# Rows gathered per job by a slot table instead of scattered, and job 0 fixed to expert 0

## The reference

```python
def reference(...):
    x = attn(q, k, v, g_q, g_k)       # batch 4, 12 heads, 448 rows, head width 64; q and k rms-normed
    x = x.transpose(0, 2, 1, 3).reshape(1792, 768)
    xn = x / (norm(x) + 1e-6)
    en = emb / (norm(emb) + 1e-6)
    logits = xn @ en.T / tau          # 8 experts
    expert = argmax(logits, 1)
    gate = softmax(logits)[expert]
    for e in range(8):                # w1: 768 x 1024, w2: 1024 x 768 per expert
        m = expert == e
        y[m] = gate[m, None] * (relu(x[m] @ w1[e]) @ w2[e])
    return (sigmoid(y @ w_gate) * (y @ w_val)) @ w_out    # 768 x 1536, 1536 x 768
```

## Time and profile before

| | us |
|---|---|
| median of 3 runs (1240.18 to 1243.33) | 1241.68 |
| the profiled execution | 1241.44 |
| its span, first to last instruction | 1239.7 |
| TensorE (PE) busy | 1136.6 (92%) |
| VectorE (DVE) busy | 650.4 (52%) |
| ScalarE (ACT) busy | 575.0 (46%) |
| GpSimd (POOL) busy | 238.3 (19%) |
| DMA moved | 146.28 MB, mean 118 GB/s |

### The profile page before, as it was taken

How to read it: one execution, slowest core, us unless ns; L and a number is a source line. 1 busy time by engine, 2 the same in 40 slices (tenths; PEclk the granted TensorE clock), 3 DMA queues, 4 the chain that set the end, 5 groups by cost and what they waited for, 6 DMA issues and landing times. The chain is left out here.

```text
span 1239.7 us, 22058 instructions
## 1 busy us (share of the span) xinstructions
PE 1136.6 (92%) x7426; PEld 997.4 (80%) x7427; DVE 650.4 (52%) x1112; ACT 575.0 (46%) x1272; POOL 238.3 (19%) x217
## 2 busy tenths in 40 slices
PE   4999999999406999999999899999999999999995
PEld 2566666666206999999999899999999999999995
DVE  4677777776625656666566333334433333334332
ACT  3777777777004555555555333233332433233321
POOL 7576766664330000000000000010000000010001
PEclk9999999999657999999999999999999999999998
DMA  2122121212177875778765643343333533343331
GB/s 88 28 66 61 50 67 44 67 45 53 35 202 188 204 188 160 184 194 232 194 171 167 157 120 108 102 147 102 103 112 96 156 110 102 102 146 102 111 111 50
DMA packets 242678, 146.28 MB, mean 118 GB/s; under 512 B 8258, under 2 KB 237890, under 8 KB 242574
## 3 DMA queue, kind: packets, MB, share of 16 engines
q1 hardware_dynamic: 240087, 134.86, 40.1%
q0 software_dynamic: 2560, 11.02, 2.7%
HBM read 133.94 MB, written 11.92 MB: 118 GB/s over the span
## 5 line engine op out<-in xcount | busy, mean ns | idle before, releaser
L1309 POOL DMA_INDIRECT out_dram<-rows,idp x16 | 18.2, 1136 | 861.3 <-DVE rows L1271 857.6
L1262 DVE TENSOR_TENSOR gv<-vb,sg 128x448 f32<-128x448 f32 x48 | 30.0, 625 | 218.4 <-PE vb L1327 218.4
L495 ACT ACTIVATE PR<-sc,negmax 112x448 f32<-112x448 f32 x192 | 122.2, 660 | 0.0
L1104 PE MATMUL hb<-XL,W1H 128*128 128x256 f32 (+1 forms) x384 | 110.1, 287 | 7.4 <-issue 7.4
L363 DVE TENSOR_REDUCE negmax<-sc 112x2 f32<-112x896 f32 x96 | 100.8, 1087 | 28.8 <-PE sc L590 28.6
L1103 PE MATMUL hb<-XH,W1H 128*128 128x256 f32 (+1 forms) x384 | 110.3, 287 | 2.9 <-DVE W1L L1050 2.9
L1103 PE MATMUL yb<-HH,W2H 128*128 128x256 f32 (+1 forms) x384 | 112.7, 293 | 0.0
L1218 ACT ACTIVATE l_WH<-stream 128x768 fp32r<-128x768 f32 x100 | 82.2, 840 | 62.3 <-PE vb L1327 60.8
L1325 PE MATMUL gb<-YH,l_WH 128*128 x288 | 106.6, 370 | 3.9 <-DVE l_WL L1255 3.6
L1105 PE MATMUL hb<-XH,W1L 128*128 128x256 f32 (+1 forms) x384 | 109.7, 286 | 0.0
L1105 PE MATMUL yb<-HH,W2L 128*128 128x256 f32 (+1 forms) x384 | 109.4, 285 | 0.0
(11 more groups left out here) (179 smaller groups left out, 2649.8 us busy)
## 6 DMA issues: line engine op xcount, KB each, us to landing
raw<-in_moe_w_dram SPq DMA_DIRECT2D x66, 384.0 KB, 5.3
stream<-in_moe_w_dram SPq DMA_DIRECT2D x48, 512.0 KB, 4.7
stream<-in_moe_w_gate_dram SPq DMA_DIRECT2D x34, 384.0 KB, 3.5
stream<-in_moe_w_val_dram SPq DMA_DIRECT2D x34, 384.0 KB, 4.0
stream<-in_moe_w_out_dram SPq DMA_DIRECT2D x32, 384.0 KB, 3.8
xr<-x_sorted SPq DMA_DIRECT2D x9, 768.0 KB
l_raw<-in_moe_w_gate_dram SPq DMA_DIRECT2D x16, 384.0 KB, 3.5
l_raw<-in_moe_w_val_dram SPq DMA_DIRECT2D x16, 384.0 KB, 4.0
```

Source lines behind the costliest of these rows:

```text
L495: nc.scalar.activation(PR[:, h, j, :], sc[j % 2][0:P, h, 0:S], ACT.Exp, bias=negmax[:, s, j, h:h + 1], accum_out=den[:, s, h, j:j + 1]).th ...
L1104: nc.tensor.matmul(out[:, 0:n], WH[:, slot, k, :], ml, start=False, stop=False)
L1262: nc.vector.tensor_tensor(gv[:, f % 2, :], vb[f % 2][:, 0:S], sg[:, f % 2, :], ALU.mult).then_inc(prod, 1)
```

## The change

- Attention writes each pair's rows of x from a buffer of two pairs to `x_rows` in DRAM (SP, `write_x`), unscaled; the gate is written as a last column after the routing.
- SP's pipeline in attention is unrolled. During pairs 4 to 10 it also loads w1 blocks 0 to 3 and w2 blocks 0 to 2 of expert 0. ACT and DVE split the first two w1 blocks at the end of attention. Job 0 is expert 0 even when that expert has no token.
- The routing block is gone; its work is part of attention's last steps, in an early part (three batches) and a late one. A token's slot (rank within its expert) is divided by 73 into a chunk and a line. With one-hots `LO` (line, times the token's number) and `HI` (expert's chunk), sixteen products `LO x HI` sum to a table of 73 lines by 224 columns of token numbers. `early_slots` is twelve operations of 112x224 on POOL; `finish` holds the last pick, the ranks, the late `HI`, the norm, the gate and the copies of the table; `job_table` is 21 small operations. Four columns are the rows of a job.
- The last pair is mixed in another bank (`mix_bank`).
- POOL gathers a job's 4 x 73 rows by four indirect DMAs (`fetch_rows`), for job 0 at the end of attention, for the others in a loop of its own in experts, where it also scales the rows by the gate and stores the job's token numbers to `ids`.
- SP's order of loads in experts changes: four w1 blocks of the next job are loaded ahead.
- Layer 2 reads the token numbers from `ids` as integers.

```diff
 # attention, SP
-            pipeline(step, -2, 23, sp)
-            sp.wait_ge(c.consts, c.CONSTS)
-            for share in SHARES:
-                sp.dma_start(c.pad_rows[share, :], c.zeros[share, :]).then_inc(c.padded, 16)
+            for n in range(-2, PAIRS):
+                load_v(0, n + 1)
+                load_qk(0, n + 4)
+                write_x(n - 2)
+                first_weights(n - 4)
+            write_x(PAIRS - 2)
+            write_x(PAIRS - 1)
+            sp.wait_ge(r.gated, 1)
+            for b in range(B):
+                sp.dma_start(x_rows[b * S:(b + 1) * S, DM:ROW].rearrange("(p t) a -> p (t a)", t=NT),
+                             r.gate[:, b * NT:(b + 1) * NT], allow_slow_non_contiguous=True).then_inc(gate_written, 16)
 # attention, POOL
-            pipeline(step, -2, PAIRS + 2, pool, {-2: emb_norm, PAIRS - 1: lambda: constants(nc, c, pool)})
+            pipeline(step, -2, PAIRS, pool, {-2: emb_norm, 3: lambda: constants(nc, r, pool), 20: logits_early})
+            early_slots()
+            x_squares(0, PAIRS - 2)
...
+            pool.wait_ge(r.ranked_l, 1)
+            for i in range(EARLY, TILES):
+                nc.gpsimd.tensor_scalar(r.LO[:, i, :], r.lines[:, :], r.b[:, i:i + 1], r.token[:, i:i + 1],
+                                        ALU.is_equal, ALU.mult).then_inc(r.lo_l, 1)
+            for ring in range(2):
+                pool.wait_ge(x_written[ring], 16 * PAIRS // 2)
+            pool.wait_ge(gate_written, 16 * B)
+            pool.wait_ge(c.first_index, 1)
+            fetch_rows(nc, c, x_rows)
 # attention, DVE
-            pipeline(step, -1, PAIRS + 2, dve, {-1: emb_scale, 0: emb_out, PAIRS: pick_first})
+            dve_hooks = {-1: emb_scale, 0: emb_out, 21: pick_early, PAIRS - 1: early_ranks, PAIRS: early_lines}
+            pipeline(step, -1, PAIRS, dve, dve_hooks)
+            first_lows()
+            logits(0, PAIRS - 2)
+            pair_squares(0, PAIRS - 2)
+            finish()
+            job_table()
 # attention, ACT, after its pipeline
+            for f in range(2):
+                act.wait_ge(c.raw1_in[f], 16)
+                for ks in halves(KD):
+                    nc.scalar.activation(c.W1H[:, f, ks, :], c.raw1[:, f, ks, :], ACT.Copy).then_inc(c.w1_hi, 1)
+            out_T(0, PAIRS - 1)
+            for t in range(NT):
+                nc.scalar.activation(last_junk[:, t, :], X[:, (PAIRS - 1) % 2, t, :], ACT.Square,
+                                     accum_out=QP[:, PAIRS - 1, t:t + 1]).then_inc(r.last_sq, 1)
 # attention, TensorE
-            pipeline(step, -1, PAIRS + 2, pe, {0: turn_emb})
+            pipeline(step, -1, PAIRS - 1, pe, {0: turn_emb, PAIRS - 2: count_early})
+            turn_probs(0, last, 2)
+            turn_probs(0, last, 3)
+            mix(0, last - 1, 2)
+            mix(0, last - 1, 3)
+            pe.wait_ge(r.ranked_e, 1)
+            route(0, last - 2)
+            turn_rows(0, last - 1)
+            for i in range(NT):
+                mix(0, last, i)
+            route(0, last - 1)
+            index_map(range(0, 4), r.lo_e, r.hi_e)
+            turn_rows(0, last)
+            route(0, last)
+            pe.wait_ge(r.picked_l, 1)
+            count(r.OHL, sc[1][:, 0, 0:E * NT], sc[1][:, 0, E * NT:2 * E * NT], E * NT, r.counted_l)
+            index_map(range(4, EARLY), r.lo_e, r.hi_e)
+            index_map(range(EARLY, TILES), r.lo_l, r.hi_l).then_inc(r.mapped, 1)
+def fetch_rows(nc, c, x_rows):
+    for a in range(4):
+        nc.gpsimd.indirect_dma_start(out=c.xr[:, a, :], out_offset=None, in_=x_rows[:, :],
+                                     in_offset=bass.IndirectOffsetOnAxis(ap=c.index[:, a:a + 1], axis=0))\
+            .then_inc(c.x_got[a], 16)
 # experts, SP
-            n_jobs = jobs(sp)
-            load_x(0)
...
-            with sp.Fori(0, n_jobs) as j:
-                e = expert_of(sp, j)
-                load_w1(e, j, 2)
-                load_w1(e, j, 3)
-                load_x(j + 1)
-                for f in range(4, F1):
-                    load_w1(e, j, f)
-                    load_w2(e, j, f - 4)
-                for d in range(F1 - 4, F2):
-                    load_w2(e, j, d)
-                load_w1(following, j + 1, 0)
-                load_w1(following, j + 1, 1)
+            def rest_of(e, following, j):
+                for f in range(4, F1):
+                    load_w1(e, j, f)
+                load_w1(following, j + 1, 0)
+                load_w2(e, j, 3)
+                load_w1(following, j + 1, 1)
+                load_w2(e, j, 4)
+                load_w1(following, j + 1, 2)
+                load_w2(e, j, 5)
+                load_w1(following, j + 1, 3)
+            n_jobs = jobs(sp)
+            rest_of(0, expert_of(sp, 1), 0)
+            with sp.Fori(1, n_jobs) as j:
+                e = expert_of(sp, j)
+                for d in range(3):
+                    load_w2(e, j, d)
+                rest_of(e, expert_of(sp, j + 1), j)
 # experts, POOL (had nothing to do before)
+            store_ids(0)
+            pool.wait_ge(c.all_indices, 1)
+            with pool.Fori(0, n_jobs) as j:
+                pool.wait_ge(x_turned, KD * (j + 1))
+                pool.wait_ge(ids_out, 16 * (j + 1))
+                nc.gpsimd.tensor_copy(c.index[:, :], c.indices[:, bass.ds(column_of(pool, j + 1), 4)]).then_inc(index_in, 1)
+                pool.wait_ge(index_in, j + 1)
+                pool.sem_inc(x_asked, 1)
+                fetch_rows(nc, c, x_rows)
+                store_ids(j + 1)
+                for a in range(4):
+                    pool.wait_ge(c.x_got[a], 16 * (j + 2))
+                    pool.sem_inc(x_arrived, 1)
+                    scale_rows(nc.gpsimd, a).then_inc(x_in, 1)
 +        def scale_rows(eng, a):
+            return eng.tensor_scalar(xr[:, a, 0:DM], xr[:, a, 0:DM], xr[:, a, DM:ROW], None, ALU.mult)
 # experts, job 0: ACT scales quarters 0 and 2, DVE 1 and 3; TensorE turns quarter by quarter
+            for a in (1, 3):
+                dve.wait_ge(c.x_got[a], 16)
+                scale_rows(nc.vector, a).then_inc(gated_dve, 1)
```

More of the change, by code:

```diff
@@ L188, in attention @@
         x_ready = sem("x_ready")
+        x_written = [sem(f"x_written{i}") for i in range(2)]
+        gate_written = sem("gate_written")
         routed = sem("routed")
@@ new lines, in _, with best @@
+            early, late = slice(0, EARLY), slice(EARLY, TILES)
+            def best(tiles, OH):
+                LG, mx, first, fm = r.LG[:, tiles, :], r.mx[:, tiles], r.first[:, tiles, :], r.fm[:, tiles]
+                wide = [P, tiles.stop - tiles.start, E]
+                chain(nc.vector.tensor_reduce(mx, LG, AX.X, ALU.max))
+                chain(nc.vector.tensor_tensor(first, LG, mx.unsqueeze(2).to_broadcast(wide), ALU.is_ge))
+                chain(nc.vector.tensor_tensor(first, first, r.rank[:, 0:wide[1], :], ALU.mult))
+                chain(nc.vector.tensor_reduce(fm, first, AX.X, ALU.max))
+                return nc.vector.tensor_tensor(OH[:, :, :].rearrange("p e i -> p i e"), first,
+                                               fm.unsqueeze(2).to_broadcast(wide), ALU.is_equal)
@@ L641, in turn_rows @@
                 pe.wait_ge(oT_out, p + 1)
+                if mix_bank(it, n) is not av:
+                    pe.wait_ge(x_ready, p)
                 for t in range(NT):
@@ new lines, in index_map @@
+            def index_map(tiles, lo, hi):
+                for i in tiles:
+                    pe.wait_ge(lo, i % EARLY + 1)
+                    pe.wait_ge(hi, i % EARLY + 1)
+                    last = nc.tensor.matmul(sc[0][0:LINES, 1, 0:SLOTS], r.LO[:, i, :], r.HI[:, i, :],
+                                            start=(i == 0), stop=(i == TILES - 1))
+                return last
+            pipeline(step, -1, PAIRS - 1, pe, {0: turn_emb, PAIRS - 2: count_early})
+            last = PAIRS - 1
@@ L1133, in _ @@
             pe.wait_ge(banks_set, HB + YB)
-            for kd in range(KD):
-                turn(0, kd, first_banks[kd])
+            for a in range(4):
+                pe.wait_ge((gated_act, gated_dve)[a % 2], a // 2 + 1)
+                for kd in range(KD):
+                    last = nc.tensor.transpose(first_banks[kd][:, a * R:(a + 1) * R], xr[:, a, kd * 128:(kd + 1) * 128],
+                                               c.ident[0:R, 0:R])
+                    if a == 3:
+                        last.then_inc(x_turned, 1)
             with pe.Fori(0, n_jobs) as j:
@@ L1408 @@
+        layer2(nc, c, w_l2, ids, out)
 _INS = ["q", "k", "v", "g_q", "g_k", "moe_expert_emb", "moe_tau", "moe_w1", "moe_w2",
```

647 lines of the change are left out of this document (367 added, 280 removed).

## The result

The changed kernel takes **1349.88 us** (median of four runs, 1346.42 to 1352.27) against 1240.93 us for the kernel before, run beside it: a ratio of 1.0876, 95% interval 1.0841 to 1.0911. The forecast was 1222 us and 91% for faster. It is 128 us away, and on the wrong side.

A forecast was written before the change was run, and what follows sets the result against it. TensorE is nearly full except for a gap between attention and the jobs. From 1241.4 us: minus 24.9 up to the first product, minus 5.4 of issue stall, plus 11.2 in the jobs, gives 1222; range 1207 to 1234.

The forecast's parts named there:

- Inside the jobs: Eight expert jobs: GpSimd's gathers and scalings delay VectorE's weight splits by 1.4 us a job, plus 11.2, bounds 0 and 34.
- Up to the index map: End of attention: last logits at 326.9, picks, counting and twelve more index products, done at 336.1 us.
- From there to the first product: Gate, gate stores, four gathers, scaling and transposes before job 0: first product at 352.0 rather than 376.9, minus 24.9.
- The issue stall: After job 0's first matmul: 7.4 us of waiting for instructions behind loads falls to 2, minus 5.4.
- the stall stays: Rival, after job 0's first matmul: instruction fetch takes its time whatever the DMA does; 1227.7 us, chance 0.13.
- TensorE needs them at 439: in time: Job 1's rows: gathers and id store issued from 417.6, scalings from about 424.8 to 429, before TensorE needs them.
- Their start ... id store 1.2: GpSimd's sequence for job 1's rows from 417.6: register load and index copy 0.9, gathers 5.1, id store 1.2 us.
- SP's order of loads keeps four W1 blocks ahead, which only helps: SyncE's weight loads in the jobs: the new order was taken as harmless and given no cost.
- The hold-up: In the jobs, VectorE's two-SBUF-input subtractions wait for GpSimd's scalings of 0.98 us each: 1.4 us a job, 11.2 in all.
- The slower rival: In the jobs, scalings of 1.32 us block VectorE in full, 4.3 us a job, 34.4 in all: 1245.5 us, chance 0.07.

The follow-up runs named there:

- B alone: Changed kernel with the store of token numbers issued by SyncE in one piece of 73 lines instead of by GpSimd: 1342.67 us, ratio 1.082.
- C alone: Changed kernel with SyncE's weight loads in the order of the kernel before: 1363.94 us, ratio 1.0993.
- D after A alone: Changed kernel with gathers of 80 rows, and ScalarE scaling the rows instead of GpSimd: 1282.93 us, ratio 1.0336.
- e6: Changed kernel with gathers of 80 rows and token numbers stored by SyncE in shares of 64 and 9 lines; GpSimd scales: 1258.94 us, ratio 1.0139.
- e7: e6 with ScalarE scaling the rows instead of GpSimd: 1254.48 us, ratio 1.0111.
- e1: Changed kernel with each gather widened from 73 to 80 rows, the extra rows unused: 1272.88 us, ratio 1.0254.
- e14: Changed kernel with gathers of 80 rows, numbers in shares by SyncE and SyncE's load order of before; GpSimd scales, gathers early: 1239.12 us, ratio 0.9983.
- e3: Changed kernel with gathers of 80 rows and token numbers stored by SyncE in one piece of 73 lines: 1284.18 us, ratio 1.0349.
- e9: e7 with SyncE's loads in the order of the kernel before and the store of numbers moved behind w2 block 4: 1237.72 us, ratio 0.9985.
- e12: e11 with GpSimd scaling the rows again instead of ScalarE: 1257.85 us, ratio 1.0151.
- e11: e7 with gathers asked after block 0 of the job, ScalarE's scalings moved along, and SyncE's load order of before: 1247.15 us, ratio 1.0077.
- e13: e9 with ScalarE's four scalings placed after blocks 5 and 6 instead of 4 and 5: 1245.69 us, ratio 1.0037.
- e10: e7 with gathers asked after block 0 of the job and ScalarE scaling after blocks 5 and 6: 1301.49 us, ratio 1.0493.
- e2: Changed kernel, gathers still of 73 rows, with SyncE storing the token numbers in one piece of 73 lines: 1342.67 us, ratio 1.082.

## Why the prediction was wrong

The loss by cause, each step measured on top of the one before it:

| version | us | step |
|---|---|---|
| the change | 1349.9 | |
| gathers of 80 rows (A) | 1272.9 | -77.0 |
| numbers in shares by SyncE (B) | 1258.9 | -14.0 |
| SyncE's order of before, with the store later (C) | 1239.1 | -19.8 |
| ScalarE scales (D) | 1237.7 | -1.4, within the noise |

The steps are in this order only: B alone was worth 7 us, C alone -14, D after A alone -10, D after A and B 4.5 (e6 to e7). Of the 77 us, 11.6 lie ahead of the first product; the rest, the 14 and the 20 us are what the sum lacked in the part "Inside the jobs"; the fourth, which it had, was nearly nothing.

- **Up to the index map: nearly right.** Forecast 336.1. The cast of the first index is at 337.66; attention was not slowed, and POOL's constants were hidden.

```profile
337.66 0.16 DVE L707 CAST index<-sc 73x4 uint32<-73x4 f32 x1 [3.61 <-PE sc L1003]
...
338.43 0.32 DVE L712 CAST indices<-sc 73x224 uint32<-73x224 f32 x1
```

- **From there to the first product: 19.7 us too early** (352.0 for 371.65), in four terms. This is the timeline of GpSimd and then of ScalarE and TensorE, answering to the earlier trace rows:

```profile
343.98 2.11 POOL L1047 DMA_INDIRECT xr<-x_rows,index  x1 [8.85 <-issue]
346.39 1.83 POOL L1047 DMA_INDIRECT xr<-x_rows,index  x1 [0.30 <-issue]
...
350.65 1.81 POOL L1047 DMA_INDIRECT xr<-x_rows,index  x1 [0.30 <-issue]
```

```profile
364.42 1.76 ACT L1252 ACTIVATE xr<-xr 73x768 f32<-73x768 f32 x2 [30.02 <-PEq L189]
...
365.50 0.48 PE L1363 MATMUL tx<-ident,xr 73*128 73x73 f32 x2 [27.87 <-ACT xr L1252]
...
371.65 0.58 PE L1329 MATMUL hb<-XH,W1H 128*128 128x256 f32 x1 [3.00 <-DVE XL L1284]
```

The gathers begin at 343.98 for 341.9 (+2.1). Issuing takes 8.5 for 5.1 (+3.4); the price of a scatter's issue was carried over to a gather, and in e1, with 80 rows, it would have been right (0.9 and a gap of 0.3). From the last issue to the next block it is 11.7 us for 3.3 (+8.4): the landing was taken from a load of 7 KB, while the four gathers move 900 KB; with 80 rows it is 4.0 us (348.4 to 352.4 in e1), inside the stated bound of 6.3. And from the block's start to the product it is 7.5 for 1.7 (+5.8). The prediction names a scaling of 0.67, six transposes of 0.15 and parts of 0.43 and 0.45; that is 2.45 us, and 1.7 has only one transpose in it. Each of the four quarters has six, 24 in 3.15 us, and the parts XH and XL of six banks follow one another. That last one is an error of counting, and owes nothing to the hardware. It stays when the gather is repaired: in e1 the first product is 8.0 us later than forecast, and 5.9 of it lie there.

- **The issue stall: not relieved.** It was 7.4 us before and forecast at 2. It is 4.8 here, later in the jobs, and 8.7 in two places in e14, one of them ahead of the first product. What was won at one place came back at another, and the rival "the stall stays" was nearer. The reading that the DMA's load delays the instructions is not refuted by that: e3 and e6 differ in one store alone, and the stall ahead of the first product is 11.8 us in the one and 5.2 in the other. Emptier queues as such did not remove it, though.

- **"TensorE needs them at 439: in time" is the step that failed.** The landing was not worked out at all there: between the last issue and the first scaling the sum has no term for it. With 21 us to landing (12.5 with nothing else running) and 2.4 us a scaling, the rows of job 1 came 19.5 us late, and the w1 blocks came late as well (67.0 us of waits). Eighty rows in place of 73, and nothing else, give back 77 of the 109 us that the change lost.

- **"Their start ... id store 1.2": the store was mis-sized, and only as an issue.** Its issue is 2.9 us, and the DMA engines pay about 3 us more with next to no bytes moved. The prediction asked what small elements cost for the gate stores, where it turned out to be little (4-byte packets of 8 ns, landing 2.4 us at the median), and not for the one store that was expensive.

- **"SP's order of loads keeps four W1 blocks ahead, which only helps": true of the change as it was, by 14 us, and false once the gather is repaired**, by 17 to 20 us together with the place of the store. What it buys in blocks 0 to 3 it seems to take from blocks 4 to 7.

- **The hold-up: the mechanism was right, the size was wrong both ways.** VectorE does wait for GpSimd. The rule cited from the Trainium skill (SBUF — State Buffer, SBUF: two separate sides), that the loser of the shared ports is blocked, is borne out for the half that was open: 0.4 us on W2L and 1.3 on a pair of W1L. No row shows a block as long as a scaling. A scaling is 2.4 us, not 0.98. But of 6.8 us held up, at most 1.4 arrive against e9, not 11.2. That is with the rows early; with the rows late GpSimd's scalings cost 10.7 us in all (e12).

- **The gain was there, and is given back.** In e14 the first product starts at 362.57, 14.3 us before. From there to the end it is 874.7 us against 862.8. Of these 11.9, 8.0 are waits for W1L, and 3.5 are saved on issue (3.9 for 7.4 behind the first product). The rest is in the matmuls. The jobs as stretches, of e14 and then of the kernel before, and then the stretch of e14 behind its second stall:

```profile
362.50:402.50 40.00, 39.67 (x323) 39.23 (x324) 23.94 (x47) 19.95 (x47) 17.32 (x14) 0.95 0.62 156
402.50:680.00 277.50, 265.05 (x2176) 261.35 (x2174) 168.13 (x336) 143.67 (x337) 91.08 (x59) 0.99 0.75 182
```

```profile
376.90:417.00 40.10, 32.70 (x271) 32.63 (x272) 18.72 (x39) 17.06 (x40) 0.00 (x0) 0.86 0.65 170
417.00:683.00 266.00, 264.78 (x2228) 264.57 (x2226) 168.53 (x346) 146.98 (x345) 0.00 (x0) 1.00 0.73 191
```

```profile
486.00:489.00 3.00, 3.00 (x16) 3.00 (x15) 0.00 (x0) 0.00 (x0) 1.88 (x2) 0.50 1.14 230
```

The same 2499 matmuls keep TensorE busy for 304.7 us instead of 297.5, beside 12.8 us of idle time instead of 8.6. The clock explains a small part. In the jobs of the kernel before, TensorE is busy at the lower of its two clock levels only behind the first matmul, up to 388 us; in e14 it is so for 3.9 us behind the first product, and for 3 us more behind the stall of 3.9 us that ends at 485.65. Counted at half speed, that is some 1.6 us of the 7.2, an estimate from these stretches. Most of the rest lies in the products of h, which read W1H and W1L (high by high 294 ns for 284 on the mean, and 290 for 289 in the products of y). That they wait for an operand in their midst would fit, and is not shown. So a repaired kernel ends level with the old one: many waits of up to 1.1 us, and slower matmuls, take back what the shorter gap had won.

The slower rival had the right sign and the wrong mechanism: even a complete hold-up was worth 1245.5. No rival had a transfer that runs on one DMA engine of sixteen, so no chance was given to what happened, and the range ended at 1234.

## What to carry to other kernels

Before pricing any transfer, factorise its row count: 73 or 76 rows to a gather is 77 or 23 us here against 80, at fewer bytes, and splitting 73 into 64 and 9 was already in the code that the change took out. A landing time is a price for its own shape and size, so take it from a row of the same kind or write down how many bytes per engine it stands for. And after a repair, run the discarded rivals again: the order of before cost 14 us before the gather was mended, and won 17 to 20 after it, with the store moved along. Last, change one thing at a time: e11 seemed to price late gathers at 9.4 us, until e13 showed that the scalings moved with them cost about as much alone.

## What the runs showed of the hardware that was not expected

- A gather by GpSimd of 73 rows of 3 KB: 1.83 us to issue, 540 additional packets of 8 bytes, 12.5 us to landing with no other transfer under way, 51 GB/s for four. Of 80 rows: 0.91 us, none, 3.6 to 9.5 us, 164 GB/s.
- A store of 292 four-byte elements by GpSimd kept the DMA engines 87% busy for 4 us at 12 GB/s. By SyncE in shares of 64 and 9 lines it takes 1.3 us of issue, and the kernel is 14 us faster. Why the packets of the one are 256 bytes and 0.7 us long and those of the other 4 bytes and 8 ns stays open.
- A product of 73x768 by a scalar per line takes GpSimd 2.4 us and VectorE 0.61 (two in 1.15), 3.1 against 0.8 ns an element of a line.
- The same gathers, asked some 8 us later, cost 18.7 us where GpSimd scales (e12 against e14), some 1.5 us and within the noise where ScalarE does (e11 against e13), and 47 us in the other order of loads, there with the scalings moved too (e10 against e7). Only in e10 did the landing get longer (14.7 for 8.3 us at the median); why was not separated.
- TensorE's clock fell to its lower level behind waits of 3.9 us (e14, 0.50 from 486 to 489 us) and of 7.1 us (the change, 0.66 from 445 to 455 us).
- A store in one piece of 73 lines ahead of the first product goes with a stall of 11.8 us there (e3; 11.2 in e2), the same store in shares of 64 and 9 with one of 5.2 us (e6).
